# Splitting the first weights of the MoE layer up to two turns later, and loading retention chunks three in flight

## The reference

```python
scores = scale * np.matmul(q, k.transpose(0, 1, 3, 2))
ret = scores * Dmat[None, :, :, :]          # gamma ** (i - j) for i >= j, else 0
x = np.matmul(ret, v)                       # -> 1152 tokens x 512 features
p = domain_probs / (domain_probs.sum(-1, keepdims=True) + 1e-09)
for e in range(E):                          # 4 experts, w1 512 x 1024, w2 1024 x 512
    h = np.maximum(x @ w1[e], 0.0)
    out += p[:, e:e + 1] * (h @ w2[e])
h = out @ w_in                              # 512 x 2048
g = h * np.tanh(softplus(h))
return g @ w_out                            # 2048 x 512
```

## Time and profile before

| | before |
|---|---|
| median of 3 runs | 626.48 us |
| the profiled execution | 627.09 us |
| its span | 625.2 us |
| TensorE busy | 618.1 us (99%) |
| GpSimd, VectorE, ScalarE busy | 285.0, 271.6, 237.0 us |
| HBM read | 47.45 MB |

### The profile page before, as it was taken

One profiled execution on the slowest core, in us unless ns is written; L12 is line 12 of the kernel. 1 busy time (PEld: TensorE's weight loads), 2 busy tenths in 40 slices (PEclk: granted clock), 3 DMA queues, 4 the chain that ended last, 5 costly groups with the idle time before them and its releaser, 6 DMA issues.

```text
span 625.2 us, 9507 instructions
## 1 busy us (share of the span) xinstructions
PE 618.1 (99%) x3773; PEld 553.7 (89%) x3773; DVE 271.6 (43%) x388; ACT 237.0 (38%) x459; POOL 285.0 (46%) x239
## 2 busy tenths in 40 slices
PE   8999999999999999999999999999999999999997
PEld 5788899999999999999999899988989999989996
DVE  5646854433154433154433154434545432324334
ACT  3446423432223432123442223435455454334431
POOL 4657645553435542535543635532435553443300
PEclk9999999999999999999999999999999999999999
DMA  8955312332102321212312212321211233201002
GB/s 271 318 185 174 106 48 68 101 89 63 51 35 68 102 79 57 68 35 67 102 67 69 69 35 67 88 81 35 68 34 35 68 117 85 68 0 52 1 0 102
DMA packets 25147, 50.43 MB, mean 81 GB/s; under 512 B 2896, under 2 KB 3216, under 8 KB 25104
## 3 DMA queue, kind: packets, MB, share of 16 engines
q1 hardware_dynamic: 24816, 49.66, 25.4%
q10 hardware_dynamic: 288, 0.17, 0.1%
HBM read 47.45 MB, written 2.36 MB: 80 GB/s over the span
## 4 chain that ended last, share of the span: by engine, by line
PE 97%; DMA 1%; DVE 1%; issue 0%; ACT 0%; SPq 0%; DVEq 0%; ACTq 0%
PE bank L494 31%; PE bank L496 30%; PE bank L495 30%; PE bank L448 2%; PE bank L488 2%; DMA qkv<-in_chunks 1%; PE bank L619 1%; PE bank L452 1%; PE bank L626 0%; DVE acc_sb L895 0%; DVE acc_sb L899 0%; ACT qkv L696 0%; DVE qkv L822 0%; DVE h_lo L856 0%; SPq L418 0%
## 5 line engine op out<-in xcount | busy, mean ns | idle before, releaser
L395 POOL TENSOR_TENSOR w_lo<-w_raw,w_hi 128x512 fp32r<-128x512 f32 x96 | 132.2, 1389 | 150.7 <-ACT w_hi L368 148.9
L494 PE MATMUL bank<-w_hi,h_hi 128*128 128x512 f32 x432 | 168.8, 391 | 0.0
L496 PE MATMUL bank<-w_hi,h_lo 128*128 128x512 f32 x432 | 168.4, 390 | 0.0
L495 PE MATMUL bank<-w_lo,h_hi 128*128 128x512 f32 x432 | 168.3, 390 | 0.0
L882 DVE TENSOR_TENSOR h_act<-part,bank 128x384 f32<-128x384 f32 x96 | 52.9, 552 | 169.7 <-PE bank L496 168.9
L390 POOL TENSOR_TENSOR ws<-ws_f,ws 128x1024 fp32r<-128x1024 f32 x24 | 57.6, 2400 | 145.1 <-ACT ws L364 145.1
L496 PEld LDWEIGHTS bank<-w_hi,h_lo 128*128 128x128 f32 x432 | 81.1, 188 | 16.9
L495 PEld LDWEIGHTS bank<-w_lo,h_hi 128*128 128x128 f32 x432 | 81.1, 188 | 12.3
L494 PEld LDWEIGHTS bank<-w_hi,h_hi 128*128 128x128 f32 x432 | 81.0, 188 | 12.2
L732 ACT ACTIVATE part<-bank 128x384 f32<-128x384 f32 x72 | 35.4, 491 | 139.3 <-PE bank L496 139.3
L849 DVE SCALAR_TENSOR_TENSOR h_lo<-h_act,h_hi 128x384 fp32r<-128x384 f32 x64 | 74.3, 1170 | 20.6 <-ACT h_hi L722 20.0
(11 more groups left out here) (87 smaller groups left out, 911.4 us busy)
## 6 DMA issues: line engine op xcount, KB each, us to landing
w_raw<-in_weights SPq DMA_DIRECT2D x144, 256.0 KB, 2.8
qkv<-in_chunks SPq DMA_DIRECT2D x18, 512.0 KB, 4.6
out<-acc_sb SPq DMA_DIRECT2D x6, 256.0 KB, 2.0
out<-acc_sb SPq DMA_DIRECT2D x1, 768.0 KB, 3.6
consts<-in_consts ACTq DMA_DIRECT2D x1, 146.0 KB, 3.6
ident<-in_consts SPq DMA_DIRECT2D x1, 64.0 KB, 4.0
consts<-in_consts SPq DMA_DIRECT2D x1, 34.0 KB, 3.9
p_nat<-in_probs ACTq DMA_DIRECT2D x1, 18.0 KB, 3.6
```

The lines of the kernel that those rows point to most:

```text
L395: pool.tensor_tensor(w_lo[layer][:, x], w_raw[:, r % RAW], w_hi[layer][:, x].bitcast(F32), ALU.subtract).then_inc(s_wl, 1)
L494: pe.matmul(out, w[0], x[0], start=first, stop=False, **more)
L495: pe.matmul(out, w[0], x[1], start=False, stop=False, **more)
L496: return pe.matmul(out, w[1], x[0], start=False, stop=last, **more)
```

## The change

Three tables of the order change; no arithmetic does. First-layer units 0 to 7 are split in turns 5, 7, 9, 10, 11, 12, 13, 13 (before: 5 to 12), second-layer units 0 to 2 in turns 14, 15, 15 (before: 12, 13, 14). SyncE loads each chunk c once chunk c-3 has landed, with the weight units at the places of `WEIGHTS_WITH`. Where TensorE reads the tiles is unchanged. In the changed file lines 74 to 423 of before stand five lines further down, and from L434 on two lines further up.

```diff
+WEIGHTS_WITH = {7: 0, 9: 1, 11: 2, 12: 3, 13: 4, 14: 5, 15: 6, 16: 7, 17: 8}
+W1_IN = (5, 7, 9, 10, 11, 12, 13, 13)
@@
     for u in range(UNITS):
-        add(IN_TURN, 5 + u, "w1", 0, u)
+        add(IN_TURN, W1_IN[u], "w1", 0, u)
     for u in range(3):
-        add(IN_TURN, 12 + u, "w2", 0, u)
+        add(IN_TURN, 14 + (u + 1) // 2, "w2", 0, u)
@@
-            for c in range(2, 6):
+            for c in range(2, CHUNKS):
                 if c > 2:
                     chunk_there(c - 3)
                 load_chunk(c)
-            for u in range(UNITS):
-                chunk_there(3 + u)
-                load_weights(u)
-                chunk_there(4 + u)
-                load_chunk(6 + u)
-            for c in range(6 + UNITS, CHUNKS):
-                chunk_there(c - 3)
-                load_chunk(c)
-                load_weights(UNITS + c - 6 - UNITS)
+                if c in WEIGHTS_WITH:
+                    load_weights(WEIGHTS_WITH[c])
             sp.dma_start(ident[:, :], consts_in[:, CONSTS:]).then_inc(s_id, 16)
-            for r in range(UNITS + CHUNKS - 6 - UNITS, len(LOADS)):
+            for r in range(len(WEIGHTS_WITH), len(LOADS)):
                 load_weights(r)
```

## The result

| | before | with the change |
|---|---|---|
| median of 6 runs | 626.84 us | 647.36 us |
| lowest and highest | 626.34, 630.25 | 646.27, 650.60 |
| profiled execution | 627.09 | 646.27 |
| its span | 625.2 | 644.5 |
| TensorE busy | 618.1 | 624.3 |

The ratio is 1.0325, 95% interval 1.0293 to 1.0358: 3.3% slower, 20.5 us between the medians and 19.3 between the two profiled spans. I had forecast 639.2 and a range that ended at 645.

What follows compares the result with a forecast made beforehand. TensorE was taken as the bound, busy 618.1 of 625.2 us; waits of 10.9 plus 2.3, less 0.5, gave +12.7 us on the profiled 627.09, or 639.2 us on the median of 626.48. Range about 636 to 645.

Steps and rivals of the forecast that it cites:

- The three waits: Turns 9, 10, 11: TensorE waits for low parts of tiles 2 to 4, 3.01, 2.96 and 3.02 us, adding up.
- tile 5's 1.92: Turn 13: TensorE waits 1.92 us after the scores for the low part of tile 5, split in turn 12.
- The tail: Turn 15 to P6: sums start 2.6 us later, slack 0.32, so TensorE waits 2.3 us before P6.
- The clock: Rival: TensorE's granted clock falls to its lower level in the new waits; 644.8 us, chance 0.12.
- a wait is shorter than the work between two: Turns 9 to 13: argument against the clock falling, waits of 3 us with about 4 us of work between.
- the sum: Whole kernel: +10.9 + 2.3 - 0.5 = +12.7 us, with no term for the clock.
- a fall from the start of the program: Start: nine filler matmuls take 3.64 us against about 2.3, so some 1.4 us lost per fall.
- My rival: New waits: four falls of the clock add 5.6 us, giving 644.8 us; chance 0.12.
- The early turns: Turns 3 to 6: the new load order gains 0.5 us, bounds 0 and 1.6.
- the queue: Turn 6: 1.07 us of issue may be an instruction fetch held up by a full queue; 0.5 taken off.
- turn 7 at 0.1: Turn 7: moving tile 1 there from turn 6 costs 0, with a bound of 0.1 us.

Runs made afterwards that it cites:

- e1_split_only: The change's table of splits alone, with the loads in the order of before: 648.05 us, ratio 1.0306.
- e3_one_turn: The change, but first-layer units 2 to 5 are split one turn earlier (turns 8 to 11): 630.86 us, ratio 1.0047.
- e5_tail_only: The kernel before with second-layer units 0 to 2 split in turns 14, 15, 15, as in the change: 630.08 us, ratio 1.006.
- e12_copy_first: e3_one_turn, but ScalarE copies P1's bank before it splits second-layer units 6 and 7, not after: 628.98 us, ratio 1.0031.
- e4_fillers: The change with filler matmuls on TensorE in its waits (turns 9, 10, 11, 13 and ahead of P6): 641.13 us, ratio 1.0208.
- e7_one_wait: e3_one_turn with first-layer unit 2 back in turn 9, the turn that reads it: 636.30 us, ratio 1.0154.
- e8_every_chunk: Splits of before, chunks loaded three in flight, a weight unit behind every chunk from 7 on: 626.97 us, ratio 1.0006.
- e6: e3_one_turn, but second-layer unit 2 is split behind the sums, in turn 16: 630.93 us, ratio 1.0069.
- e2: The change's load order alone, with the splits of before: 631.31 us, ratio 1.0068.
- e11: e8_every_chunk with no filler matmuls in turn 6: 626.43 us, ratio 0.9996.
- e9: e8_every_chunk with 4 filler matmuls in turn 6 where there were 8: 628.49 us, ratio 1.0013.
- e10: The kernel before with 4 filler matmuls in turn 6 where there were 8: 626.74 us, ratio 0.9997.

## Why the prediction was wrong

**The mechanism and the waits: right.** The three waits of 3.01, 2.96 and 3.02 measured 2.97, 2.92 and 2.97, tile 5's 1.92 measured 1.89, and none was hidden. `e1_split_only` and `e3_one_turn` show that they come from the table of splits.

**The tail: right in place and size.** Two low parts more ahead of the sums make the wait, as `e5_tail_only` shows by itself; 2.3 was forecast, 2.52 measured (2.3 in `e5_tail_only`). VectorE's subtraction for chunk 16 again outlasted GpSimd's, here 79.58 and 1.95 long against 78.97 and 2.41. `e12_copy_first` confirms ScalarE's copy as what P6 waits for.

**The clock: the step that failed.** I gave the fall of the clock 0.12 and held against it that "a wait is shorter than the work between two". So the sum had nothing for the clock, and it measured 6.2 us (`e4_fillers` against the change), more than the 2.4 by which the time left the range. Nothing in the trace supported the argument: its longest idle stretch after the start was 1.1 us, and I took the silence of rows on 3 us of idle as an argument. Three waits with no cover, and a start at which the same matmuls ran at half rate, should have carried the larger part of the chance. The price was off as well. I read 1.4 for a fall from the start of the program; in the change they cost 1.5, 2.8 and 1.7, and the one in turn 9 of `e7_one_wait` 2.6. My rival reckoned four equal falls, 5.6; there were three of uneven length, together 6.0 by the timeline and 6.2 by `e4_fillers`, which is close to that sum by luck. Even the rival's 644.8 falls 2.6 short, since it shared the two terms below.

**The early turns: a gain that no run shows.** I took 0.5 off for the queue and bounded it by 1.6. `e8_every_chunk` puts three chunks in flight at 1.0006 of before, which leaves room for a gain of 0.8 us at most: the bound is refuted, the 0.5 is neither shown nor excluded. I also misread the new order, in which unit 0 still goes behind chunk 7, so there is a load of weights among chunks 6 to 8. The gap in turn 6 differs from run to run in all kernels; the 1.4 us that the change seemed to win there against the one trace of before was two executions compared, and I carried that error into the expectations of three experiments.

**A small wait unforeseen.** Turn 7's 0.9: VectorE's low part of chunk 5 took 1.26 beside two decays of v on GpSimd, and tile 0 waits for it. I had bounded turn 7 at 0.1, by tile 1 alone. The two decays run one behind the other because turn 6 holds no split any more. The wait (0.6 to 1.4 us) stands in the traces of the change, e1, e4, e6 and e12, which all have that table and a gap of 0.2 to 0.3 in turn 6. It is missing in e3 and e7, which have the table and a gap of 1.1 and 1.6, and in e2, which has the small gap and the splits of before. So in these traces it takes both, the table and a TensorE that comes early into turn 7; no run varied the gap on purpose.

With the clock's 6.2, the early 0.5 taken back and turn 7's 0.6 to 0.9, the forecast of 639.2 becomes 646.5 to 646.8, against 647.36. The forecast stood on a median of 626.48, and the six runs of before have 626.84, which is 0.36 of what is left.

## What to carry to other kernels

Before a producer's step is moved later, find the consumer on the bound engine and the chain between: here a split behind the turn's own output takes 2.9 us, and one turn of lead is all that it needs. A new wait of some microseconds on TensorE is to be priced at the wait plus up to as much again for the clock; filler matmuls in the wait took that second part away. Here a load order that feeds an engine which did not wait for loads bought nothing that could be measured, and it cost 4 us when the table of who reads them was not moved with it.

## What the runs showed of the hardware

- The low clock behind a wait of 2 to 3 us is not certain, and length alone does not decide it: the same wait of 3.0 in turn 9 left the clock at 1.00 in the change and at 0.51 for 7 us in `e7_one_wait`, and the wait before P6 gave mean clocks of 1.000 and of 0.997 in executions of one kernel (`e5_tail_only`). In turn 6 it fell behind gaps of 1.95 (e11), 2.17 (e8) and 2.40 (e9) and not behind 2.13 (e10). Behind 1.5 before P6 it did not fall in any of 9 runs (`e12_copy_first`). It makes such kernels scatter: the change ran from 646.27 to 650.60, the first with a mean clock of 0.989, the last with 0.982.
- Elementwise differences of 768 columns on VectorE take 0.94 to 0.96 us alone and 2.04 to 2.05 beside GpSimd's low parts of weights.
- TensorE has an idle gap of 0.2 to 2.4 us in turn 6 with no releaser that explains it, in every trace; where it is over 1 us, a 16 KB instruction packet lands 1.3 to 1.8 us before it ends. Runs of e8 to e11 lie in groups 2 to 3 us apart; that the gap makes the groups is not shown.
